# An attention-and-two-layer kernel on one core: a tile's low part ahead of the next pair's decay, and the first pair of unit 1 a step sooner

## The reference, cut to what matters

```
state = zeros(B, H, D, D)                       # B=4, H=8, S=768, D=48
for t in range(S):
    state = alpha[:, :, t, :, None] * state + einsum('bhd,bhe->bhde', k[:, :, t], v[:, :, t])
    y[:, :, t] = einsum('bhd,bhde->bhe', q[:, :, t], state)
x = y as (3072 tokens, 384)
x = square(relu(x @ moe_w_in)) @ moe_w_out      # 384 -> 2048 -> 384
out = silu(x @ moe2_w_in) @ moe2_w_out          # 384 -> 2048 -> 384
```

## Time and profile before

| | before |
|---|---|
| median of 3 runs (us) | 926.88 (925.53 to 929.38) |
| the profiled execution, its own time (us) | 928.33 |
| its span in the profile (us) | 926.7 |
| mean granted clock of PE | 0.985 |
| PE busy | 891.9 us, 96% |
| DVE busy | 416.4 us, 45% |
| ACT busy | 399.6 us, 43% |
| POOL busy | 66.2 us, 7% |
| PE waiting for `x_lo` (4 times) | 21.1 us |
| PE waiting for `y_sb` (once) | 1.8 us |

### The profile page before, as it was taken

How to read it: one execution, slowest core, us unless ns; L and a number is a source line. 1 busy time by engine, 2 the same in 40 slices (tenths; PEclk the granted TensorE clock), 3 DMA queues, 4 the chain that set the end, 5 groups by cost and what they waited for, 6 DMA issues and landing times.

```text
span 926.7 us, 17305 instructions
## 1 busy us (share of the span) xinstructions
PE 891.9 (96%) x6906; PEld 729.9 (79%) x6906; DVE 416.4 (45%) x907; ACT 399.6 (43%) x710; POOL 66.2 (7%) x97
## 2 busy tenths in 40 slices
PE   7999889989997999799999999999999999999997
PEld 6777668767786888687888888888888888888897
DVE  7588856674776676565243411311312212212310
ACT  4765544444444444443566633323323323323520
POOL 2453200000000000001023100000000000000000
PEclk9999979998998999999999999999999999999999
DMA  9985415233322334221043200110200200100100
GB/s 156 225 221 118 103 32 135 63 77 82 78 64 63 97 70 93 56 70 44 17 147 103 86 35 0 43 26 1 58 12 0 69 1 23 47 0 1 35 11 28
DMA packets 106233, 60.02 MB, mean 65 GB/s; under 512 B 56416, under 2 KB 99808, under 8 KB 106144
## 3 DMA queue, kind: packets, MB, share of 16 engines
q1 hardware_dynamic: 100784, 51.84, 23.2%
q0 software_dynamic: 2048, 6.29, 2.2%
q10 hardware_dynamic: 3312, 0.69, 0.6%
HBM read 45.02 MB, written 9.44 MB: 59 GB/s over the span
## 4 chain that ended last, share of the span: by engine, by line
PE 91%; DVE 5%; issue 2%; ACT 1%; DMA 1%; ACTq 0%; DVEq 0%; POOL 0%
PE h_ps L840 41%; PE z_ps L854 38%; PE jobs L872 3%; PE jobs L715 1%; PE jobs L817 1%; DVE decay L1252 1%; PE jobs L748 1%; PE jobs L825 1%; PE jobs L726 1%; DVE decay L1239 1%; PE z_ps L872 1%; DVE kp L1211 1%; DMA nat_k<-in_k 1%; PE jobs L704 1%; PE h_ps L654 0%
## 5 line engine op out<-in xcount | busy, mean ns | idle before, releaser
L1355 DVE TENSOR_TENSOR g_lo<-g,g_hi 128x512 fp32r<-128x512 f32 x177 | 122.4, 692 | 355.1 <-ACT g_hi L1073 243.0
L840 PE MATMUL h_ps<-x_hi,win_hi 128*128 128x512 f32 x576 | 228.4, 397 | 22.0 <-DVE x_lo L1347 21.1
L840 PE MATMUL h_ps<-x_hi,win_lo 128*128 128x512 f32 x576 | 225.4, 391 | 0.0
L840 PE MATMUL h_ps<-x_lo,win_hi 128*128 128x512 f32 x576 | 225.1, 391 | 0.0
L1068 ACT ACTIVATE g<-h_ps 128x512 f32<-128x512 f32 x96 | 57.4, 598 | 232.1 <-PE h_ps L840 232.1
L1070 ACT ACTIVATE g<-h_ps 128x512 f32<-128x512 f32 x96 | 57.3, 596 | 205.7 <-PE h_ps L840 205.7
L840 PEld LDWEIGHTS h_ps<-x_hi,win_hi 128*128 128x128 f32 x576 | 108.4, 188 | 47.4 <-DVE x_lo L1347 23.0
L840 PEld LDWEIGHTS h_ps<-x_hi,win_lo 128*128 128x128 f32 x576 | 108.6, 189 | 23.1
L840 PEld LDWEIGHTS h_ps<-x_lo,win_hi 128*128 128x128 f32 x576 | 108.6, 189 | 21.5
L854 PE MATMUL z_ps<-g_hi,wout_hi 128*128 128x512 f32 x288 | 118.7, 412 | 0.0
L1073 ACT ACTIVATE g_hi<-g 128x512 fp32r<-128x512 f32 x177 | 111.8, 632 | 5.6
(11 more groups left out here) (155 smaller groups left out, 840.9 us busy)
## 6 DMA issues: line engine op xcount, KB each, us to landing
z_scratch<-z_sb SPq DMA_DIRECT2D x18, 256.0 KB, 2.6
x_raw<-z_scratch SPq DMA_DIRECT2D x6, 768.0 KB, 4.5
v_sb<-in_v SPq DMA_DIRECT2D x44, 96.0 KB, 2.7
out_x<-z_sb SPq DMA_DIRECT2D x80, 48.0 KB, 1.7
nat_a<-in_alpha SPq DMA_DIRECT2D x40, 88.0 KB, 2.2
nat_k<-in_k SPq DMA_DIRECT2D x40, 88.0 KB, 2.5
nat_q<-in_q SPq DMA_DIRECT2D x40, 88.0 KB, 2.3
nat_a<-in_alpha SPq DMA_DIRECT2D x40, 80.0 KB, 2.2
```

Of the source, the lines that this page charges most:

```text
L840: last = nc.tensor.matmul(h_ps[f % 2][:], w[:, f, tile(kk)], x[par][:, kk, :], start=(kk == TILES[0] and n == 0), stop=(kk == TILES[-1] an ...
L1355: nc.vector.tensor_tensor(low, g[f % 2][:], high.bitcast(F32), ALU.subtract).then_inc(g_lo_made, 1)
```

## The change

In four places. First, DVE and ACT split the last tile of x for units 2 to 5 at f = 14 together with the other two, no longer at f = 15. For unit 1 the last tile stays at f = 15, but on DVE it now stands between the turning of pair 8's q and its multiplication, ahead of `low_g(15)` and of pair 9's decay (`q_turn` is taken out of `q_stage` for this). Second, pair 4: KQ at F = 2 instead of 3, S at 4, I at 4 instead of 5, Y at 5 instead of 6. Third, its backward scan stands ahead of `low_g(0)` and its growth behind it. Fourth, on PE every S now stands between the products and every I behind them, and pair 4's jobs on DVE take the order of the other pairs.

```
-        return {"A": 1, "KQ": 3, "S": 4, "I": 4 + (n == PAIRS), "Y": 5 + (n == PAIRS)}[kind] + 3 * (n - PAIRS)
+        return {"A": 1, "KQ": 2 if n == PAIRS else 3, "S": 4, "I": 4, "Y": 5}[kind] + 3 * (n - PAIRS)
 def behind(kind, n):
-    return kind == "S" and n == PAIRS or kind == "I" and n > PAIRS
+    return kind == "I"
 # ACT
-                if f == SPLIT_STEP + 1 and u + 1 < UNITS:
+                if f == SPLIT_STEP + (u == 0) and u + 1 < UNITS:
                     split_x_last((u + 1) % 2, u + 1)
 # DVE
+            def q_turn(n):
+                turn("q", n, q_turned)
+
             def q_stage(n):
                 early = n < PAIRS
-                if not early:
-                    turn("q", n, q_turned)
...
                         if n != 2 * PAIRS:
+                            q_turn(n)
                             q_stage(n)
+                if F == 0:
+                    a_scan(PAIRS)
                 if F == stage_step("KQ", 2 * PAIRS) + 1:
+
+                    q_turn(2 * PAIRS)
+                    split_x(1, 1, TILES[-1:])
                     q_stage(2 * PAIRS)
-
-                if F == stage_step("I", PAIRS):
-                    decay_stage(PAIRS)
-                    i_stage(PAIRS)
-                    a_scan(PAIRS + 1)
-                    a_grow(PAIRS + 1)
                 low_g(u, f, g_pair(F), u >= UNITS, NF * u)
                 if F == 0:
-                    a_scan(PAIRS)
-                if F == 1:
                     a_grow(PAIRS)
-                if F == stage_step("A", PAIRS + 1):
-                    a_turn(PAIRS + 1)
                 for kind, n in jobs_here:
-                    if kind == "I" and n > PAIRS:
+                    if kind == "I":
                         decay_stage(n)
                 for kind, n in jobs_here:
-                    if kind == "A" and n > PAIRS + 1:
+                    if kind == "A" and n > PAIRS:
                         a_turn(n)
                 for kind, n in jobs_here:
-                    if kind == "I" and n > PAIRS:
+                    if kind == "I":
                         i_stage(n)
                 for kind, n in jobs_here:
-                    if kind == "A" and n > PAIRS + 1:
+                    if kind == "A" and n > PAIRS:
                         a_scan(n)
                         a_grow(n)
...
-                if f == SPLIT_STEP and u + 1 < UNITS:
-                    split_x(u + 1, (u + 1) % 2, TILES[:-1])
-                if f == SPLIT_STEP + 1 and u + 1 < UNITS:
-                    split_x(u + 1, (u + 1) % 2, TILES[-1:])
-                if f == SPLIT_STEP and UNITS <= u + 1 < 2 * UNITS:
-                    split_x(u + 1, (u + 1) % 2)
+                if f == SPLIT_STEP and u + 1 < 2 * UNITS:
+                    split_x(u + 1, (u + 1) % 2, TILES[:-1] if u == 0 else TILES)
```

## The result

The changed kernel takes 900.62 us in the median (899.96 to 901.81), the kernel before 927.12 over its four runs. The ratio is 0.9714 with a 95% interval of 0.9691 to 0.9737, so it is faster by 26.5 us, 24.4 to 28.7 by the interval. Forecast was 30.7 less, 896.2, with a range of 892.0 to 902.5. The profiled execution took 899.96 with a span of 898.4 us, 28.3 us less span than the one before.

The account below looks back on a forecast made before the run. PE, busy 96% of the span, was taken as the bound, so only its waits and slow-clock work could yield time. 22.16 us at units 2 to 4 plus 8.5 at unit 1 (2.2 pair 4's) gave 30.7 less: 896.2, range 892 to 902.5.

Parts of the forecast that it names:

- the big term: At units 2 to 4, splitting the last tile of x at f = 14 saves 22.16 us.
- the place to which the stall moves: At unit 1, PE newly waits about 3.5 us for `kt_copy` ahead of I of pair 8.
- The forecast case: Whole kernel 30.7 us less, 896.2 us, with the clock staying at 2.4 GHz; chance 0.47.
- the fallen clock: At unit 1, the clock also falls at the new wait: 2.7 us less gain, 898.9 us; chance 0.28.
- Units 2, 3 and 4, 22.16 us: All excess at these boundaries, slow matmuls included, goes: 8.13 + 7.32 + 6.71 us.
- Pair 4, 2.2 us: In steps 0 to 7, PE's waits of 1.82 us ahead of S of pair 5 and about 0.25 us go.
- the prediction's way of counting: For PE's waits, the point where work could start is 0.16 us ahead of the idle time shown.
- DVE and POOL slow each other: One possible reason why pair 4's part gives nothing: 2.2 us less gain, 898.4 us; that rival's chance 0.12.
- Unit 1: Step 17 starts at 119.1 instead of 127.64: 8.5 us gained, of which 2.2 are pair 4's.
- The clock: At unit 1's new wait, the clock was taken as staying at 2.4 GHz over 3.5 us of waiting.
- The first rival: At unit 1, the clock falls at the new wait too: 2.7 us less gain, 898.9 us; chance 0.28.
- 4.8 us of idle time were just enough: At unit 4's wait the clock was granted at 1.00 throughout, so 3.5 us may not make it fall.

Follow-up runs that it names:

- POOL held back: Changed kernel, with POOL making its last two of 7 early low weights only once pair 4's scan is made: 898.06 us, run again 900.0 us.
- the run with that wait ahead of S of pair 9: Changed kernel with pair 9's scans and growth moved behind pair 8's state: 900.35 us, ratio 0.9712.
- `y_stage` ahead of `low_g(17)`: Changed kernel with POOL's last two early weights delayed, pair 9's scans behind pair 8's state, its decay check two steps later, pair 8's `y_stage` ahead of `low_g(17)`: 896.64 us.

## Why the prediction was right

The time fell inside the range and the direction was right: the big term and the place to which the stall moves were foreseen. The forecast case itself did not come. The gain forecast, 30.7 us, was above the interval's 24.4 to 28.7; against the spans, 28.3, it is 2.4 too large. It is the room that the range left for the fallen clock and for pair 4 that holds 900.62. By its own terms:

- **Units 2, 3 and 4, 22.16 us:** the trace gives 21.6, the part alone 21.1 (19.3 to 23.0). To take each boundary from the point where the tile could have started to the next product at full clock, and not the wait alone, was what got it. The moved decay was in no one's way: S of pair 13 followed its product.
- **Pair 4, 2.2 us:** 1.66. Mis-sized. The step that failed is that the scan moved ahead of `low_g(0)` "takes some 1.8 us [...] and lies in an idle time of 3.25 us": it took 3.74 without the inversion, since POOL was working beside it, and made PE wait 0.40 us for `low_g(0)`, 0.56 with the 0.16 us of the prediction's way of counting. That is all that is missing: where POOL held back, the gain was 28.37 - 26.10 = 2.27 us. I had read the scan's duration from rows where POOL had stopped, and did not look at what POOL did in the place it was moved to. "DVE and POOL slow each other" stood among the rivals, with 0.12, but at nothing in the sum.
- **Unit 1:** the stall went where it was said to go, ahead of I of pair 8, 3.2 us for the 3.5 forecast, and 0.4 us for the 0.54 at the tile. Step 17 came 7.97 us sooner for 8.5, and the 0.5 missing are those of pair 4.
- **The clock:** the forecast took it as staying, with 0.47, against 0.28 for its fall at a price of 1.7 to 3.6 us. It fell, and cost 1.54, a little less than the least price. The first rival was the case that came, together with the smaller gain at pair 4. It should have been the forecast: the clock had fallen at all four waits of before, and it fell in all nine runs of the changed kernel. The chance rested on one of those four, at which the clock was still full when the work came back, read as "4.8 us of idle time were just enough". The clock can fall when the wait is over, so that row does not show this, and in the run with the later units' tile alone 1.8 us were enough.
- The sum closes: 30.7, less 0.5 for pair 4, 1.54 for the clock, 0.24 for the head and 0.5 at units 2 to 4, and 0.5 more behind them, is 28.4, the 28.3 of the spans. The medians lie 1.8 us nearer to each other than the spans. Step 2 starts at 36.9 to 39.1 in the profiles of this study, so a single profile's span carries about 2 us that no edit made.

Not settled: what decides whether the clock falls behind a wait of 2 to 3 us. The same kernel did both.

## What to carry to other kernels

Ask of each thing on a helper engine's list who waits for it first: a tile of 0.67 us stood behind 5 us of work that nobody needed yet, and each wait for it, 5 us, cost 6.7 to 8.1 us by the prediction's count with the slow clock behind it (21.6 us for three, as measured). When such a wait is removed, look for the next result behind the same long piece of work, and for every engine that waits for that piece in its own order; moving it alone moved the wait without shortening it. And time a moved instruction by its new neighbours: the same scans took twice as long beside GpSimd.

## What the runs showed of the hardware

The clock of TensorE fell not only during a wait but also after work had begun again, 1.4 us after it in the changed kernel, where PE went on at 119.24: it was 1.00 in 115.0 to 119.3, 0.90 in 119.3 to 121.0 and 0.50 in 121.0 to 123.4. It fell behind a wait of 2.4 us in the one profile with it, behind 3.2 us in five profiles of seven and in the run with that wait ahead of S of pair 9 (a second product of 3.78 us). Behind a wait of 1.8 us it fell in one profile (the later units' tile alone) and did not in three (the kernel before, unit 1's tile alone, `y_stage` ahead of `low_g(17)`). Those shorter waits cost 1.5 to 2.8 us on top of themselves.

A scan of 112x64 on DVE took 0.26 us in the median and up to 1.05 us with POOL at work beside it. Eight took 1.56 us with POOL idle, 2.17 with one of its instructions beside them and 3.74 with three.
